# Trial operations on four engines in front of a fused attention and channel-mix kernel

## The reference

```
q_pool = q.reshape(B, H, S // 2, 2, D).mean(axis=3)
scores = (1 / sqrt(D)) * q_pool @ k.T;  attn = softmax(scores)
x = (attn @ v) as (B, S // 2, H * D)
xn = (x - mean) / sqrt(var + 1e-6) * g_ln
out = x + relu(xn @ w_ch1) @ w_ch2
```

## Time and profile before

| | us |
|---|---|
| median of 2 runs | 862.64 |
| lowest, highest | 860.82, 864.46 |
| the profiled execution | 864.73 |
| its span, first to last instruction | 862.9 |
| TensorE busy | 818.7 |
| VectorE busy | 504.4 |
| GpSimd busy | 358.2 |
| ScalarE busy | 330.7 |

### The profile page before, as it was taken

One profiled execution on the slowest core, in us unless ns is written; L12 is line 12 of the kernel. 1 busy time (PEld: TensorE's weight loads), 2 busy tenths in 40 slices (PEclk: granted clock), 3 DMA queues, 4 the chain that ended last, 5 costly groups with the idle time before them and its releaser, 6 DMA issues.

```text
span 862.9 us, 15883 instructions
## 1 busy us (share of the span) xinstructions
PE 818.7 (95%) x6564; PEld 687.6 (80%) x6564; DVE 504.4 (58%) x683; ACT 330.7 (38%) x695; POOL 358.2 (42%) x248
## 2 busy tenths in 40 slices
PE   6799999999899999989989999999999999999998
PEld 3676777667777667777769999999999999999997
DVE  5689999999999999998625543213223123222111
ACT  1455656556575556565543341121111111121110
POOL 1468899999778788777780000000000000000000
PEclk7699999999999999999999999999999999999999
DMA  5846355533465533530103321001001001001001
GB/s 117 182 102 145 95 120 136 137 89 87 100 136 137 125 79 89 119 82 29 49 30 98 122 73 37 1 1 37 1 1 37 1 1 38 1 0 37 1 1 37
DMA packets 30807, 58.51 MB, mean 68 GB/s; under 512 B 8208, under 2 KB 18704, under 8 KB 27152
## 3 DMA queue, kind: packets, MB, share of 16 engines
q1 hardware_dynamic: 29520, 56.90, 26.4%
q10 hardware_dynamic: 1216, 0.59, 0.3%
HBM read 52.76 MB, written 4.72 MB: 67 GB/s over the span
## 4 chain that ended last, share of the span: by engine, by line
PE 67%; POOL 18%; DVE 8%; ACT 3%; issue 3%; DMA 1%; POOLq 0%; SPq 0%; ACTq 0%; DVEq 0%
PE banks L957 23%; PE banks L970 23%; POOL acc L401 15%; PE banks L528 7%; PE banks L539 4%; POOL acc L405 3%; PE banks L475 3%; DVE pm L745 2%; PE banks L526 2%; ACT pT L651 2%; DVE kT L710 2%; PE banks L555 2%; DVE qT L722 1%; PE banks L247 1%; DMA k_in_rows<-in_k_dram 1%
## 5 line engine op out<-in xcount | busy, mean ns | idle before, releaser
L401 POOL TENSOR_TENSOR acc<-acc,pT 128x576 f32<-128x576 f32 x160 | 237.3, 1483 | 24.7 <-ACT pT L651 1.8
L957 PE MATMUL banks<-xT,weights 128*128 128x384 f32 x1152 | 217.1, 338 | 0.0
L1026 DVE SCALAR_TENSOR_TENSOR hT<-banks,hT 128x384 fp32r<-128x384 f32 x96 | 53.5, 558 | 271.4 <-ACT hT L1007 271.4
L970 PE MATMUL banks<-weights,hT 128*128 128x512 f32 x864 | 210.6, 389 | 0.0
L957 PEld LDWEIGHTS banks<-xT,weights 128*128 128x128 f32 x1152 | 202.1, 188 | 6.0 <-issue 0.2
L651 ACT ACTIVATE pT<-banks 128x576 f32<-128x576 f32 x288 | 172.1, 653 | 47.3 <-PE banks L526 41.3
L970 PEld LDWEIGHTS banks<-weights,hT 128*128 128x128 f32 x864 | 160.9, 188 | 26.8
L1007 ACT ACTIVATE hT<-banks 128x384 fp32r<-128x384 f32 x96 | 47.3, 492 | 323.3 <-PE banks L957 323.3
L745 DVE TENSOR_REDUCE pm<-banks 128x2 f32<-128x1024 f32 x128 | 153.3, 1222 | 29.5 <-PE banks L475 27.5
L528 PE MATMUL banks<-qT,kT 64*128 64x288 f32 x1728 | 163.2, 299 | 3.9 <-DVE kT L730 1.6
L528 PEld LDWEIGHTS banks<-qT,kT 64*128 64x128 f32 x1728 | 135.4, 186 | 18.7 <-DVE pm L745 6.7
(11 more groups left out here) (83 smaller groups left out, 551.0 us busy)
## 6 DMA issues: line engine op xcount, KB each, us to landing
q_in_rows<-in_q_dram SPq DMA_DIRECT2D x56, 284.0 KB, 5.6
k_in_rows<-in_k_dram SPq DMA_DIRECT2D x56, 284.0 KB, 5.1
vn<-in_v_dram SPq DMA_DIRECT2D x16, 576.0 KB, 5.2
wstage<-in_moe_w_ch_dram SPq DMA_DIRECT2D x32, 256.0 KB, 2.8
out_dram<-x SPq DMA_DIRECT2D x16, 256.0 KB, 2.1
k_in_rows<-in_k_dram SPq DMA_DIRECT2D x4, 288.0 KB, 4.9
q_in_rows<-in_q_dram ACTq DMA_DIRECT2D x2, 256.0 KB, 5.0
q_in_rows<-in_q_dram SPq DMA_DIRECT2D x2, 256.0 KB, 4.0
```

What stands on the lines that cost most here:

```text
L401: nc.gpsimd.tensor_tensor(total, pT[:, h % 2, 0] if kt == 1 else total, pT[:, h % 2, kt], ALU.add).then_inc(chained, 1)
L957: last = nc.tensor.matmul(ps_h[f % 2][:, 0:CW], weights[:, 2 * f, a, c * 128:(c + 1) * 128], xT[:, par, b, c], start=m == 0, stop=m == len ...
L970: last = nc.tensor.matmul(ps_y[kk], hT[:, f % 2, a, kk * 128:(kk + 1) * 128], weights[:, 2 * f + 1, b], start=f == 0 and m == 0, stop=f == ...
L1026: nc.vector.scalar_tensor_tensor(out=hT[:, f % 2, 1], in0=ps_h[f % 2][:, 0:CW], scalar=0.0, in1=hT[:, f % 2, 0].bitcast(f32), op0=ALU.max, ...
```

## The change

Five semaphores are added, and four functions that are called at the start of the streams. The program behind them is unchanged.

- `trial_vector` is the first thing on VectorE, ahead of line 808. It fills 2304 elements a partition of pT (half 0) with 0.5, waits, and runs two passes of nine operations, each of which waits for the one ahead: six transposes of 32 x 32 blocks (contiguous; with its output 4 elements apart; with its input in runs of 32 out of 64; contiguous into PSUM; into PSUM with its output 4 elements apart; contiguous from PSUM), two subtractions and a reduction. A six-element memset with the second count of trial_filled stands ahead of the second pass.
- `trial_gpsimd` stands after GpSimd's wait for the first count of zeros_made. It waits for the second count of trial_filled and does ten additions of 576 elements, each waiting for the one ahead.
- `trial_tensor` stands ahead of the warm-up: it waits for the eighteenth operation and does sixteen matmuls with 64 columns of weights and 128 moving columns into banks 2 and 3. TensorE then waits for ScalarE's ten and GpSimd's ten operations before the warm-up.
- `trial_scalar` stands after the loads of queries. It waits for the eighteenth operation and for the sixteen matmuls, and does ten multiplications of 64 elements out of PSUM.

```diff
--- before.py
+++ after.py
@@ -209,6 +209,8 @@
         end_turned, end_taken, sums_inv = sem("end_turned"), sem("end_taken"), sem("sums_inv")
         o_turned, x_written = sem("o_turned"), sem("x_written")
         w_hi, w_ready, early_hi, early_ready = sem("w_hi"), sem("w_ready"), sem("early_hi"), sem("early_ready")
+        trial_filled, trial_dve, trial_pool, trial_pe, trial_act = (sem("trial_filled"), sem("trial_dve"),
+                                                                    sem("trial_pool"), sem("trial_pe"), sem("trial_act"))
         stats_ready, moments_ready, var_ready, rstd_ready = (sem("stats_ready"), sem("moments_ready"),
                                                              sem("var_ready"), sem("rstd_ready"))
         xn_ready, xn_turned, xt_hi, xt_ready = sem("xn_ready"), sem("xn_turned"), sem("xt_hi"), sem("xt_ready")
@@ -373,6 +375,7 @@
             nc.gpsimd.memset(minus_half[:], -0.5).then_inc(half_made, 1)
             pool.wait_ge(half_made, 1)
             pool.wait_ge(zeros_made, 1)
+            trial_gpsimd(pool)
 
             def next_queries(j):
 
@@ -593,8 +596,85 @@
             elif kind == "T":
                 turn_tokens(0, 0, n, pair_banks("T", n)[:, 0])
 
+        def trial_source():
+            return pT[:, 0].rearrange("p t s w -> p (t s w)")
+        def trial_result():
+            return pT[:, 1].rearrange("p t s w -> p (t s w)")
+        def trial_vector(dve):
+            src, dst = trial_source(), trial_result()
+            nc.vector.memset(src[:, 0:2304], 0.5).then_inc(trial_filled, 1)
+            dve.wait_ge(trial_filled, 1)
+            wide = flat(banks[:, 0:2])
+            count = 0
+            for busy in range(2):
+                if busy:
+                    nc.vector.memset(stats[:, 0], 0.0).then_inc(trial_filled, 1)
+                nc.vector.transpose(dst[:, 0:1152], src[:, 0:1152]).then_inc(trial_dve, 1)
+                count += 1
+                dve.wait_ge(trial_dve, count)
+                nc.vector.transpose(dst[:, 0:1152].rearrange("p (t r i) -> p t i r", t=9, r=32),
+                                    src[:, 0:1152].rearrange("p (t i c) -> p t i c", t=9, c=32)).then_inc(trial_dve, 1)
...
+                nc.vector.transpose(dst[:, 0:1152].rearrange("p (t c) -> p t c", c=32),
+                                    src[:, 0:2304].rearrange("p (t c) -> p t c", c=64)[:, :, 0:32]).then_inc(trial_dve, 1)
...
+                nc.vector.transpose(wide, src[:, 0:1024]).then_inc(trial_dve, 1)
...
+                nc.vector.transpose(wide.rearrange("p (t r i) -> p t i r", t=8, r=32),
+                                    src[:, 0:1024].rearrange("p (t i c) -> p t i c", t=8, c=32)).then_inc(trial_dve, 1)
...
+                nc.vector.transpose(dst[:, 0:1024], wide).then_inc(trial_dve, 1)
...
+                nc.vector.tensor_tensor(dst[:, 0:1152], src[:, 0:1152], src[:, 1152:2304], ALU.subtract).then_inc(trial_dve, 1)
...
+                nc.vector.tensor_tensor(dst[:, 0:1024], wide, src[:, 0:1024], ALU.subtract).then_inc(trial_dve, 1)
...
+                nc.vector.tensor_reduce(dst[:, 0:18], src[:, 0:576].rearrange("p (b c) -> p b c", c=32), AX.X,
+                                        ALU.add).then_inc(trial_dve, 1)
...
+        def trial_gpsimd(pool):
+            src, dst = trial_source(), trial_result()
+            pool.wait_ge(trial_filled, 2)
+            for n in range(10):
+                nc.gpsimd.tensor_tensor(dst[:, 1152:1728], src[:, 0:576], src[:, 576:1152], ALU.add).then_inc(trial_pool, 1)
+                pool.wait_ge(trial_pool, n + 1)
+        def trial_scalar(act):
+            act.wait_ge(trial_dve, 18)
+            wide = flat(banks[:, 2:4])
+            act.wait_ge(trial_pe, 1)
+            for n in range(10):
+                nc.scalar.mul(trial_result()[:, 2304 + n * 64:2368 + n * 64], wide[:, n * 64:n * 64 + 64],
+                              trial_source()[:, n:n + 1]).then_inc(trial_act, 1)
+        def trial_tensor(pe):
+            pe.wait_ge(trial_dve, 18)
+            src = trial_source()
+            pe.wait_ge(ident_made, 3)
+            for n in range(16):
+                half = slice(n % 2 * 64, n % 2 * 64 + 64)
+                last = nc.tensor.matmul(flat(banks[:, 2:4])[half, n // 2 * 128:(n // 2 + 1) * 128],
+                                        src[:, n * 64:(n + 1) * 64], ident[:], start=True, stop=True)
+            last.then_inc(trial_pe, 1)
         def attention_tensor(pe):
             pe.wait_ge(ident_made, 3)
+            trial_tensor(pe)
+            pe.wait_ge(trial_act, 10)
+            pe.wait_ge(trial_pool, 10)
             for _ in range(WARM_UP):
                 nc.tensor.transpose(banks[:, 7, 0:128], ident[:], ident[:])
             pe.wait_ge(zeros_made, 2)
@@ -679,6 +759,7 @@
 
             act.wait_ge(zeros_made, 1)
             load_queries(act, 0)
+            trial_scalar(act)
             act.wait_ge(zeros_made, 2)
             act.wait_ge(ones_made, 3)
             for kind, n, _ in first_steps():
@@ -805,6 +886,7 @@
                 nc.vector.tensor_tensor(acc_end[:], pT[:, h % 2, KT - 2], pT[:, h % 2, KT - 1],
                                         ALU.add).then_inc(end_added, 1)
 
+            trial_vector(dve)
             nc.vector.memset(qn[REST:128, FULL], 0.0).then_inc(zeros_made, 1)
             nc.vector.memset(mx[:], 0.0)
             nc.vector.memset(q_rest[:].bitcast(f32), 0.0)
```

## The result

The changed kernel takes 899.95 us (two runs, 898.89 and 901.02) where the kernel before takes 862.64: the ratio is 1.0433, with a 95% interval of 1.0324 to 1.0541. It is slower by 37.3 us. The forecast was 906.0 with a range of 900.0 to 915.5, so the direction was right and the time fell 0.05 us under the range. Profile against profile the span went from 862.9 to 899.3, 36.4 us more, where the sum had 41.4.

A forecast was written before the change was run, and what follows sets the result against it. TensorE was busy 95% of the span, every stage waiting for the one ahead, so new work at the start shifts everything: 41.4 us on the profiled 864.73 gave 906.1, stated as 906.0, range 900 to 915.5.

The forecast's parts named there:

- the sum: Serial start costs added up: end of line 457's work moves from 10.83 to 52.2, so 41.4 us more.
- The last rival: Later in the program, idle time takes up the shift, so not slower: 866 to 880 us, chance 0.02.
- the mark: End of line 457, the last key tile's transpose, which all later work waits for: 10.83 us before, 52.2 forecast.
- its trial: VectorE's memsets and two nine-operation passes at the start: 28.7 us, from 0.90 to 29.6.
- release to mark: TensorE's warm-up, first key transposes, then queries and last key tile, with no wait between: 6.25 us.
- the doubt on the transposes: Uncertain price of VectorE's new transposes, held to be all upwards; given as reason for forecasting 906.0.
- trial five: VectorE's fifth transpose of each pass, into PSUM with output 4 elements apart: 2.10 us, no less than 1.22.
- Everything behind it has the same order and loads; no other term.: After line 457's end, the rest of the program keeps its length, adding nothing to the 41.4 us shift.
- Rival 2: TensorE's high clock lasts through the following stretch: up to 3 us back behind, 2.4 ahead of the mark; 900.7, chance 0.10.
- the likeliest case: The forecast as worked out, all new pieces in series at the start: range 903 to 908.5 us, chance 0.50.
- the contiguous transposes: Four of VectorE's six transposes per pass, writing consecutively: 1.36 us for 1152 elements, 1.22 for 1024, the lower end.
- the rival at 913.5: All VectorE trial transposes cost 1.87 ns an element, scattered or not: 7.4 us more, 913.5, chance 0.36.

The follow-up runs named there:

- e1: Changed kernel with GpSimd's ten adds moved ahead of its wait for zeros_made, so they start with VectorE's second pass: 893.12 us, ratio 1.0318 to the kernel before.
- e2: Changed kernel without GpSimd's ten adds and TensorE's wait for them: 894.09 us, ratio 1.0334 to the kernel before.
- e8: Kernel before with 34 discarded warm-up transposes in place of 16 and four more behind each of the first seven coarse scores: 865.99 us, ratio 1.0017.
- e7: Changed kernel run again, not a line altered: 902.53 us, ratio 1.0418 to the kernel before.
- e6: Kernel before run again, not a line altered: 865.68 us, ratio 1.0005.
- e9: Changed kernel with eighteen other VectorE operations, testing distances in PSUM and work beside GpSimd's released adds: run once, span 894.8 us, no ratio drawn.
- e5: Changed kernel with VectorE's second pass replaced by nine transpositions and copies in SBUF at various element distances: run once, span 899.9 us, no ratio drawn.
- e10: Kernel before with 34 discarded warm-up transposes at the start in place of 16, nothing else: 862.26 us against 865.20, ratio 0.9977.
- e3: Changed kernel with 76 more discarded transposes on TensorE between its sixteen matmuls and its waits: 897.4 us, ratio 1.0392 to the kernel before.

## Why the prediction was right and where it was wrong

**Right: the order.** All pieces stand in series, the adds do not run beside the second pass (they begin at 28.60, and e1 shows what it is like when they do), they set TensorE's release, and ScalarE is next. It was done 8.7 us earlier (e2) and not 3.5: the sum took 7.6 us for the sixteen matmuls, at their slowest, and 3.7 for the multiplications, and they took 3.60 and 2.15. The last rival, a slack that takes up the shift, is out: behind the mark there are 848 to 853 us whatever stands in front (e8 apart).

**Sizes.** Term by term, profile against profile:

| term | predicted | measured | difference |
|---|---|---|---|
| VectorE begins | 0.90 | 1.33 | +0.4 |
| its trial | 28.7 | 26.7 | -2.0 |
| from there to TensorE's release | 16.35 | 16.0 | -0.3 |
| release to mark | 6.25 | 5.7 | -0.6 |
| behind the mark, against before, by the device times | 0 | -2.6 | -2.6 |

Together 5.1 us, which is 906.1 less the profiled run's 901.02; the median of the two runs lies another 1.1 lower. Seen by the medians, the shift was 37.3 us where the sum had 41.4, and 2.1 more come from adding the sum to the profiled run, 864.73, and not to the median, 862.64. The reason given for that, that the doubt on the transposes was all upwards, was wrong for trial five.

**The failed step is "Everything behind it has the same order and loads; no other term."** The order was the same, the clock was not: 2.6 us came back behind the mark. Rival 2 had up to 3 us there, but that the figures are close is luck. It put them into the stretch that was low before from 10 to 25, and that stretch stayed low: the second key transposes took 1.97 us after as before. The 2.6 came from a later one. And I held the clock to be a thing that one kernel has and the other hasn't, with 0.10. The runs show that the changed kernel has it in one execution and not in the next (849.5 and 851.8). It belonged into the range of the likeliest case, downwards by 2.5. "TensorE: Matmul & The Clock Gate" of the Trainium skill, section "Part 1: The HAM clock gate", says that how much of a start runs at the low level varies from run to run of one kernel; the traces agree at the start itself: the same eight key transposes of the changed kernel took 1.57 us in one execution and 1.04 in the other (e7). Two runs on either side can't average it out. In the later runs the kernels were 37.5 us apart (902.53 and 865.07), and there the changed kernel's median lies inside the range that the first measurement missed by 0.05 us: which side of the bound it fell on was chance. The sum was too long all the same.

**The mis-sized term is trial five.** "Trial five does the same into PSUM: 2.34 - 128 x 1.87 ns = 2.10 us": it took 1.26, twice 0.84 less. That is 1.7 of the 2.0 us by which VectorE's trial was too long, and it is there in every run, while the share of the clock changes: between the two later profiles, e6 and e7, 38.3 us lie in front of the mark and 1.1 come back behind it. A price read in SBUF was carried to PSUM, which e9 shows not to have it. The sentence by which both pages of the Trainium skill lead to 906.1 makes the same step: what it takes from "SBUF — State Buffer" is said of SBUF. The lower bound of the term, 1.22, was in the range, but only as a side remark, and it fell on the same side as the clock: both together left the range.

**Right by the weighing: the contiguous transposes.** Taken at 1.36 and 1.22, they took 1.38 and 1.26; the rival at 913.5 falls. The rule of the Trainium skill's "Vector Engine (DVE) Microarchitecture Reference", section "3.8 The reshape front-end and per-opcode configuration", one element per cycle per lane, fits e5 in so far as a transposition took 1.04 ns an element, what a reduction takes by the earlier trace rows; how long a cycle is no run shows. That each access to a new 16-byte line pays a penalty, in the Trainium skill's "SBUF — State Buffer", section "Door 1: The DMA port swizzle", agrees with e5's 2.19 us at 4 float32 apart (16 bytes) and 0.76 at 2 apart.

**Smaller ones.** The adds came 1.48 us apart and not 1.55. Line 401 waits on two semaphores for each addition and the trial on one; that this is the reason is argued, not shown. One add met the query sum and took 2.08 in place of 1.41, 0.67 where I took 0.5:

```profile
31.56 1.41 POOL pT L652
...
33.04 2.08 POOL pT L652
```

The query transposes ran at the high level, 0.71 us in place of 1.30, and the first key transposes half at the low one, 1.57 in place of 1.07.

## What to carry to other kernels

Work put in front of a program whose stages all wait for one another cost its full chain here, less only what the clock gave back; find that chain by the order of waits in the code, as a semaphore that is given late can undo an overlap that the text of a change suggests. Take a price only from a row with the same memory on the same side of the operation: scattered in SBUF and scattered in PSUM are different prices. Where a profile shows TensorE's clock at the low level in a stretch that is bound by TensorE, what it costs there is an uncertainty of every later run, and belongs into the range of the likeliest case.

## What the runs showed of the hardware that was not expected

- On VectorE a copy of 1152 float32 that read or wrote SBUF 4 elements apart took 2.2 us, and so did a transposition that wrote so; 2 apart it took what the contiguous form does (0.76 and 1.38). In PSUM 2 to 16 apart made no difference (1.26 for 1024).
- A contiguous copy of 1152 took 0.76 us free and 1.85 beside GpSimd's adds, 2.4 times as long; a contiguous transposition kept its 1.38.
- The granted clock fell while TensorE was kept busy with transposes and coarse scores (e8), while with eighteen more discarded transposes at the very start, and none later, the median was 2.9 us lower (e10).
- The granted clock on record read 1.00 from 1 to 5 us while sixteen transposes took 3.67 us, nearly twice their 1.94 of e3.
- One and the same program took 899.2 and 902.7 us on one chip. Its two profiled executions differ by the stretch 22 to 29 us behind the mark, at 1.00 and 0.51; for the others that reason is likely, not shown.
